# Starting addresses of four pairs of moving operands, relative to the stationary ones, in a fused attention and two-MLP kernel

## The chip, the cores and the metric

The kernel runs on one core of a Trainium2 chip. The metric is the device time of one execution in microseconds (us). Each core has a TensorE for matrix products (PE in the profile, with its weight loads shown apart as PEld), a VectorE (DVE), a ScalarE (ACT), a GpSimd (POOL) and queues that issue DMAs (SP is the one used most here). All of them work out of an on-chip memory with 128 partitions; products land in a second memory with banks of 512 float32 columns per partition.

## The reference

Three blocks follow each other, with B = 2, N = 6016, C = 256:

```python
qn = q / (norm(q, axis=1) + 1e-6);  kn = k / (norm(k, axis=1) + 1e-6)
a = softmax(kn.transpose(0, 2, 1) @ qn / tau)          # 256 x 256 per batch
x = (v @ a).reshape(12032, 256)
x = (sigmoid(x @ w_gate) * (x @ w_val)) @ w_out        # width 1536
h = x @ w_in2
out = (h - tanh(h)) @ w_out2                           # width 2048
```

## The kernel before, in words

The first stage forms the 256 x 256 products of k and q over 47 blocks of 128 rows for each batch (`gram_chunk`, line 778 is its matmul), the softmax, and then folds the attention matrix into `w_gate` and `w_val`, so that v is multiplied with the folded weights and v @ a never appears by itself. Batch 0 is folded at the start (`fold_first`), batch 1 in the middle, during the one tile called SWITCH.

The second stage works through 24 tiles of tokens, 12 for each batch: 22 of 512 columns, and two (SWITCH and LAST) of 384. All operands are held transposed, so tokens are columns. Each float32 product is made of three passes with operands split in two halves named hi and lo (`product3`, line 752): w_hi with x_lo, w_lo with x_hi, w_hi with x_hi. Each pass is one weight load of 128 columns (the stationary operand, a slice of the weights) and one matmul (the moving operand, 512 or 384 columns of activations). The moving operands are four pairs:

- `vt_hi`, `vt_lo`: v transposed. `U(j)` multiplies them with `gate_w` and `val_w`: 12 matmuls for each of the J1 = 12 chunks.
- `g1_hi`, `g1_lo`: the gated product of chunk j, in 3 slots. `D(t, j)` multiplies them with `out_w`: 6 matmuls.
- `x2_hi`, `x2_lo`: the output of the first MLP. `P_(t, i)` multiplies them with `in2_w`: 6 matmuls for each of J2 = 16 chunks.
- `g2_hi`, `g2_lo`: h - tanh(h) of chunk i, in 3 slots. `O(t, i)` multiplies them with `out2_w`: 6 matmuls.

`body(t)` writes out the order on TensorE by hand: U(2) D(0) U(3) D(1) and so on up to U(11) D(9), then D(10), U(12) (which is U(0) of the next tile), D(11), U(13), then P(0) to P(3), O(0), P(4), O(1), up to P(15) O(12), and O(13) to O(15). In that order there are 49 places in a usual tile at which the moving pair changes. Waits before each step ask for product banks (`free_bank`) and for the halves (`g_lo_made`, `x2_lo_made`, `vt_lo_made`).

For each chunk ScalarE reads the bank and writes `func_out` (line 444), VectorE makes `product` (line 642 or 645), ScalarE rounds it into the hi half (line 452), and VectorE subtracts for the lo half (line 651). The vt halves come from lines 427 and 627, the x2 halves from lines 436 and 634. GpSimd splits the weights into halves at the start and once more, for gate and val, around the SWITCH tile.

`sb` allocates memory in order, each tensor at the next multiple of 32 bytes. All weights, and everything allocated before and between the four moving pairs, has a size per partition that is a multiple of 512 bytes. The slice of weights that one load reads is 128 float32, which is 512 bytes, and begins at such a multiple. So in this kernel every moving operand and every stationary operand of `product3` begins at the same place modulo 512 bytes. A 512-column moving operand reads 2048 bytes per partition.

Of the kernel before, what the change touches and what calls it, by code (L numbers as in the profile page):

```python
# [7 lines left out]
def attn_two_mlp_kernel(  # L8
# [32 lines left out]
    F32, F32R = mybir.dt.float32, mybir.dt.float32r  # L41
# [3 lines left out]
    P = 128  # L45
    B, N, C = q.shape
    KC = C // P
    J1 = w_gate.shape[1] // P
    J2 = w2_in.shape[1] // P
    T = 512  # L50
# [6 lines left out]
    SLOTS = 3  # L57
# [61 lines left out]
        return nth(t, ("U", J1 - 2 + AHEAD[tile] + i // 2), tile)  # L119

    with ExitStack() as ctx:
        def sb(name, shape, dt=F32, stack=ctx):
            return stack.enter_context(nc.sbuf_tensor(name, shape, dt))

        def sem(name):
            return ctx.enter_context(nc.semaphore(name))


        def pair(name, shape, stack=ctx):
            return sb(name + "_hi", shape, F32R, stack), sb(name + "_lo", shape, F32R, stack)  # L130

        gate_hi, gate_lo = pair("gate_w", [P, KC, J1 * P])
        val_hi, val_lo = pair("val_w", [P, KC, J1 * P])
        wout_hi, wout_lo = pair("out_w", [P, J1, C])
        win_hi, win_lo = pair("in2_w", [P, KC, J2 * P])
        wout2_hi, wout2_lo = pair("out2_w", [P, J2, C])
        att = sb("att", [P, KC, C])
        att_t_hi, att_t_lo = pair("att_t", [P, KC, C])
        ident = sb("ident", [P, P])
        ones = sb("ones", [P, P])  # L140
        v_in = sb("v_in", [P, KC, TB, Q])
# [21 lines left out]

        func_out = sb("func_out", [P, 2, T])
        product = sb("product", [P, 2, T])
        vt_hi, vt_lo = pair("vt", [P, KC, T])
        g1_hi, g1_lo = pair("g1", [P, SLOTS, T])
        x2_hi, x2_lo = pair("x2", [P, KC, T])
        g2_hi, g2_lo = pair("g2", [P, SLOTS, T])
        tau_inv = sb("tau_inv", [P, 2])  # L170


# [787 lines left out]
```

## Time and profile before

| | us |
|---|---|
| median of 2 runs | 2354.19 |
| those runs | 2353.77 and 2354.61 |
| profiled execution, its own time | 2354.47 |
| its span, first to last instruction | 2352.7 |

TensorE is at work for 98% of the span and its weight loads for 82%, VectorE 50%, ScalarE 40%, GpSimd 4%. In 38 of 40 slices the clock that TensorE was granted is at 9 tenths or more of full speed, as a mean 0.994. In the profile a matmul's duration overlaps that of the next one, since matmuls are pipelined. How fast TensorE really works is therefore read from the distance between the starts of two matmuls, called the pitch below. The printed starts are rounded to 0.01 us, so a pitch is taken over several matmuls.

### The profile page before, as it was taken

The page shows a single profiled execution, that of the slowest core. Times are in us where ns is not written, and L with a number is a line of the kernel's source. Part 1 is how long each engine was busy: PE and PEld are TensorE (multiplying, and loading weights), DVE is VectorE, ACT ScalarE, POOL GpSimd, SP SyncE. Part 2 cuts the span into 40 slices and gives each one's busy share as a digit, 9 for nine tenths or more (in the row PEclk, how much of TensorE's full clock was granted, in tenths as well). Part 3 has the DMA queues.
Part 4 walks back from the last instruction along what each step waited for, and adds up shares of the span by engine and source line. Part 5 has one row for each costly group of instructions (what it writes and reads, how often), then busy time and mean ns, then how long its engine had stood idle before and what let it go on. Part 6 is the DMA issues. An engine that isn't in the chain of part 4 may idle for free.

```text
span 2352.7 us, 28301 instructions
## 1 busy us (share of the span) xinstructions
PE 2310.6 (98%) x10332; PEld 1935.0 (82%) x10332; DVE 1166.5 (50%) x1643; ACT 935.6 (40%) x1550; POOL 105.3 (4%) x76
## 2 busy tenths in 40 slices
PE   8899999999999999999989999999999999999998
PEld 6678888888888888888888888888888888888888
DVE  6975445445354454454554544544545445445454
ACT  4544334344344343343433433434434434334343
POOL 3450000000000000000030000000000000000000
PEclk9899999999999999999999999999999999999999
DMA  8720100100100001001110010010010000100000
GB/s 294 234 63 10 18 9 9 18 9 9 18 9 9 9 9 18 9 7 18 27 45 9 8 18 9 9 18 9 9 18 9 9 10 8 18 9 7 9 9 8
DMA packets 211649, 61.81 MB, mean 26 GB/s; under 512 B 200224, under 2 KB 200480, under 8 KB 211616
## 3 DMA queue, kind: packets, MB, share of 16 engines
q1 hardware_dynamic: 208304, 49.31, 9.4%
q0 software_dynamic: 3312, 12.06, 1.7%
q8 instruction: 20, 0.33, 0.1%
q14 instruction: 13, 0.11, 0.0%
HBM read 49.02 MB, written 12.32 MB: 26 GB/s over the span
## 4 chain that ended last, share of the span: by engine, by line
PE 93%; issue 2%; DVE 2%; POOL 1%; SPq 1%; ACT 1%; DMA 1%; DVEq 0%; ACTq 0%
PE up L752 54%; PE acc L752 22%; PE x_acc L752 17%; DMA qk_in<-in_k 1%; DVE sq_sum L536 1%; POOL in_w_lo L382 0%; PE x_acc L778 0%; POOL out_w_lo L382 0%; SPq L304 0%; DVE g_lo L651 0%; SPq L294 0%; ACT squares L399 0%; POOL in_w_hi L380 0%; DVE vt_lo L627 0%; POOL out_w_hi L380 0%
## 5 line engine op out<-in xcount | busy, mean ns | idle before, releaser
L444 ACT ACTIVATE func_out<-up 128x512 f32<-128x512 f32 (+1 forms) x672 | 396.1, 589 | 827.8 <-PE up L752 827.5
L651 DVE TENSOR_TENSOR g_lo<-product,g_hi 128x512 fp32r<-128x512 f32 (+1 forms) x672 | 470.7, 701 | 391.8 <-ACT g_hi L452 389.4
L452 ACT ACTIVATE g_hi<-product 128x512 fp32r<-128x512 f32 (+1 forms) x672 | 418.5, 623 | 442.2 <-PE acc L752 216.2
L642 DVE TENSOR_TENSOR product<-up,func_out 128x512 f32<-128x512 f32 (+1 forms) x288 | 196.2, 681 | 455.1 <-ACT func_out L444 454.8
L645 DVE TENSOR_TENSOR product<-up,func_out 128x512 f32<-128x512 f32 (+1 forms) x384 | 261.2, 680 | 183.7 <-ACT func_out L444 174.8
L752 PE MATMUL up<-x_lo,in_w_hi 128*128 128x512 f32 (+1 forms) x768 | 296.6, 386 | 1.0 <-DVE x_lo L634 1.0
L752 PE MATMUL up<-x_hi,in_w_lo 128*128 128x512 f32 (+1 forms) x768 | 296.1, 386 | 0.0
L752 PE MATMUL up<-x_hi,in_w_hi 128*128 128x512 f32 (+1 forms) x768 | 296.0, 385 | 0.0
L752 PE MATMUL acc<-g_hi,out_w_hi 128*128 128x512 f32 (+1 forms) x768 | 295.4, 385 | 0.0
L752 PE MATMUL acc<-g_lo,out_w_hi 128*128 128x512 f32 (+1 forms) x768 | 295.4, 385 | 0.0
L752 PE MATMUL acc<-g_hi,out_w_lo 128*128 128x512 f32 (+1 forms) x768 | 295.3, 385 | 0.0
L752 PE MATMUL x_acc<-g_lo,out_w_hi 128*128 128x512 f32 (+1 forms) x576 | 222.3, 386 | 6.4 <-DVE g_lo L651 6.4
L752 PE MATMUL up<-vt_lo,gate_w_hi 128*128 128x512 f32 (+1 forms) x576 | 222.8, 387 | 5.7 <-issue 3.3
L752 PE MATMUL up<-vt_hi,gate_w_hi 128*128 128x512 f32 (+1 forms) x576 | 222.5, 386 | 0.0
L752 PE MATMUL up<-vt_hi,gate_w_lo 128*128 128x512 f32 (+1 forms) x576 | 222.5, 386 | 0.0
L752 PE MATMUL up<-vt_lo,val_w_hi 128*128 128x512 f32 (+1 forms) x576 | 222.1, 386 | 0.0
L752 PE MATMUL up<-vt_hi,val_w_hi 128*128 128x512 f32 (+1 forms) x576 | 222.0, 385 | 0.0
L752 PE MATMUL up<-vt_hi,val_w_lo 128*128 128x512 f32 (+1 forms) x576 | 222.0, 385 | 0.0
L752 PE MATMUL x_acc<-g_hi,out_w_hi 128*128 128x512 f32 (+1 forms) x576 | 221.9, 385 | 0.0
L752 PE MATMUL x_acc<-g_hi,out_w_lo 128*128 128x512 f32 (+1 forms) x576 | 221.9, 385 | 0.0
L752 PEld LDWEIGHTS up<-x_lo,in_w_hi 128*128 128x128 f32 x768 | 144.7, 188 | 29.6 <-issue 1.8
L752 PEld LDWEIGHTS up<-x_hi,in_w_lo 128*128 128x128 f32 x768 | 144.8, 189 | 27.5
(122 smaller groups left out, 2307.7 us busy)
## 6 DMA issues: line engine op xcount, KB each, us to landing
v_in<-in_v SPq DMA_DIRECT2D x176, 64.0 KB, 2.2
out_rows<-out_sb SPq DMA_DIRECT2D x176, 64.0 KB, 1.8
qk_in<-in_q SPq DMA_DIRECT2D x29, 384.0 KB, 4.1
qk_in<-in_k SPq DMA_DIRECT2D x29, 384.0 KB, 5.4
w_stage<-in_moe_w_out POOLq DMA_DIRECT2D x4, 512.0 KB, 4.4
w_stage<-in_moe_w_gate POOLq DMA_DIRECT2D x3, 512.0 KB, 5.1
out_sb<-in_moe_w_val POOLq DMA_DIRECT2D x3, 512.0 KB, 4.4
out_sb<-in_moe_w_out POOLq DMA_DIRECT2D x3, 512.0 KB, 4.3
```

The source lines that it names most:

```text
L444: act.activation(func_out[:, half, cut], src[:, cut], func).then_inc(func_made, 1)
L452: act.activation(hi[:, i % SLOTS, cut], product[:, half, cut], ACT.Copy).then_inc(g_hi_made, 1)
L536: dve.tensor_tensor(sq_sum[:, which, 0:size, :], sq_sum[:, which, 0:size, :], squares[:, which, 0:size, :], ALU.add).then_inc(sq_added, 1)
L642: dve.tensor_tensor(product[:, half, cut], up[2 * (i % 2) + 1][:, cut], func_out[:, half, cut], ALU.mult).then_inc(prod_made, 1)
L645: dve.tensor_tensor(product[:, half, cut], up[i % 4][:, cut], func_out[:, half, cut], ALU.subtract).then_inc(prod_made, 1)
L651: dve.tensor_tensor(lo[:, i % SLOTS, cut], product[:, half, cut], hi[:, i % SLOTS, cut].bitcast(F32), ALU.subtract).then_inc(g_lo_made, 1)
L752: mm = pe.matmul(psum, a, b, start=start and n == 0, stop=stop and n == 2, skip_group_check=shared_bank)
```

## The change

The allocator helper takes an alignment, small pads are allocated ahead of the four pairs, and three of the pairs are placed with an alignment of 4 bytes. No instruction is added, removed or moved.

```diff
-        def sb(name, shape, dt=F32, stack=ctx):
-            return stack.enter_context(nc.sbuf_tensor(name, shape, dt))
+        def sb(name, shape, dt=F32, stack=ctx, align=32):
+            return stack.enter_context(nc.sbuf_tensor(name, shape, dt, align_bytes=align))
...
-        def pair(name, shape, stack=ctx):
-            return sb(name + "_hi", shape, F32R, stack), sb(name + "_lo", shape, F32R, stack)
+        def pair(name, shape, stack=ctx, align=32):
+            return (sb(name + "_hi", shape, F32R, stack, align),
+                    sb(name + "_lo", shape, F32R, stack, align))
...
         product = sb("product", [P, 2, T])
-        vt_hi, vt_lo = pair("vt", [P, KC, T])
-        g1_hi, g1_lo = pair("g1", [P, SLOTS, T])
+        sb("pad_vt", [P, 2])
+        vt_hi, vt_lo = pair("vt", [P, KC, T], align=4)
+        sb("pad_g1", [P, 2], align=4)
+        g1_hi, g1_lo = pair("g1", [P, SLOTS, T], align=4)
+        sb("pad_x2", [P, 44], align=4)
         x2_hi, x2_lo = pair("x2", [P, KC, T])
-        g2_hi, g2_lo = pair("g2", [P, SLOTS, T])
+        sb("pad_g2", [P, 81])
+        g2_hi, g2_lo = pair("g2", [P, SLOTS, T], align=4)
         tau_inv = sb("tau_inv", [P, 2])
```

The pads are 8, 8, 176 and 324 bytes. Both halves of vt then begin 8 bytes past a multiple of 512, both of g1 16 bytes, both of x2 192 bytes, and both of g2 4 bytes (192 + 324 = 516). The weights stay where they were.

## Rows read from the trace of the kernel before

**Rows 1.** The page: busy time of each engine, share of the span, instructions.

```profile
PE 2310.6 (98%) x10332; PEld 1935.0 (82%) x10332; DVE 1166.5 (50%) x1643; ACT 935.6 (40%) x1550; POOL 105.3 (4%) x76
```

**Rows 2.** Waits of PE: who was waited for, us in total, times, longest.

```profile
PE acc L787 <- DVE expd L556: 12.7, 1, 12.7
...
PE x_acc L752 <- DVE g_lo L651: 6.4, 3, 5.5
```

**Rows 3.** Windows, PE: stretch, length, busy (matmuls), granted clock, DMA share, GB/s.

```profile
143.00:145.00 2.00, 2.00 (x6) 0.50 0.93 256
500.00:600.00 100.00, 100.00 (x443) 1.00 0.06 10
```

**Rows 4.** Groups by form, PE: count, busy us, mean ns, idle before.

```profile
L752 PE MATMUL up<-x_hi,in_w_lo 128*128 128x512 f32 x704 | 274.0, 389 | 0.0
...
L752 PE MATMUL up<-vt_hi,gate_w_hi 128*128 128x512 f32 x536 | 209.1, 390 | 0.0
...
L752 PE MATMUL x_acc<-g_hi,out_w_hi 128*128 128x512 f32 x528 | 205.5, 389 | 0.0
...
L752 PE MATMUL up<-x_hi,in_w_lo 128*128 128x384 f32 x64 | 22.1, 345 | 0.0
```

**Rows 5.** Timeline of PEld in a usual tile: start us, duration us.

```profile
1003.43 0.19 PEld L752 LDWEIGHTS x_acc<-g_hi,out_w_lo 128*128 128x128 f32 x1
```

**Rows 6.** Timeline of PE in the same stretch: first of six matmuls, and the seventh.

```profile
1003.43 0.39 PE L752 MATMUL x_acc<-g_lo,out_w_hi 128*128 128x512 f32 x1
...
1004.79 0.39 PE L752 MATMUL up<-vt_lo,gate_w_hi 128*128 128x512 f32 x1
```

**Rows 7.** Timeline of PE in the LAST tile: first of six, and the seventh.

```profile
2290.00 0.33 PE L752 MATMUL x_acc<-g_lo,out_w_hi 128*128 128x384 f32 x1
...
2291.04 0.34 PE L752 MATMUL up<-vt_lo,gate_w_hi 128*128 128x384 f32 x1
```

**Rows 8.** Timeline of PE at the start of the second stage: three pitches apart.

```profile
143.46 0.63 PE L752 MATMUL up<-vt_hi,gate_w_hi 128*128 128x512 f32 x1
...
144.74 0.63 PE L752 MATMUL up<-vt_hi,gate_w_hi 128*128 128x512 f32 x1
```

**Rows 9.** Timeline of PE in the first stage, then its group in 73 to 88.

```profile
74.75 12.47 PE L778 MATMUL x_acc<-qk_in 128*128 128x256 f32 x57
```

```profile
L778 PE MATMUL x_acc<-qk_in 128*128 128x256 f32 x69 | 15.5, 387 | 0.0
```

**Rows 10.** Timeline of PE around a fold in SWITCH: 12 matmuls of 512 columns.

```profile
1210.38 0.39 PE L752 MATMUL x_acc<-gate_w_lo,att_t_hi 128*128 128x512 f32 x1
...
1211.77 0.39 PE L752 MATMUL x_acc<-gate_w_lo,att_t_hi 128*128 128x512 f32 x1
...
1212.47 0.39 PE L752 MATMUL x_acc<-gate_w_lo,att_t_hi 128*128 128x512 f32 x1
...
1213.15 0.33 PE L752 MATMUL up<-x_lo,in_w_hi 128*128 128x384 f32 x1
```

**Rows 11.** Timeline of PE at a step from 512 to 384 columns, SWITCH.

```profile
1161.19 0.33 PE L752 MATMUL up<-vt_lo,gate_w_hi 128*128 128x384 f32 x1
...
1162.26 0.33 PE L752 MATMUL up<-vt_lo,val_w_hi 128*128 128x384 f32 x1
...
1163.30 0.33 PE L752 MATMUL x_acc<-g_lo,out_w_hi 128*128 128x384 f32 x1
```

**Rows 12.** Groups by form of the engines that write the pairs.

```profile
L651 DVE TENSOR_TENSOR g_lo<-product,g_hi 128x512 fp32r<-128x512 f32 x620 | 434.4, 701 | 365.6 <-ACT g_hi L452 363.3
L452 ACT ACTIVATE g_hi<-product 128x512 fp32r<-128x512 f32 x620 | 391.1, 631 | 405.4 <-PE acc L752 216.2 <-PE x_acc L752 132.1 <-DVE product L642 47.7
L444 ACT ACTIVATE func_out<-up 128x512 f32<-128x512 f32 x620 | 370.5, 598 | 780.1 <-PE up L752 780.1
...
L645 DVE TENSOR_TENSOR product<-up,func_out 128x512 f32<-128x512 f32 x352 | 243.4, 692 | 172.4 <-ACT func_out L444 164.4
```

## Prediction

> **What bounds the kernel now.** I began with the page's busy times: TensorE is busy for 2310.6 of 2352.7 us, and no other engine for more than half [rows 1]. The waits of TensorE come next: the longest is 12.7 us, once, in the first stage, and the longest of the second stage is 6.4 us in 3 waits [rows 2]. So about 2.2 ms are an unbroken stream of matmuls, and only their pitch, the distance from start to start, can move the time by much. A busy share near 100% does not tell whether that pitch is good, since a matmul's duration of 389 ns [rows 4] overlaps that of its neighbours.
>
> The pitch comes from windows and timelines. From 500 to 600 us 443 matmuls touch a stretch of 100 us at a granted clock of 1.00 [rows 3]; with the 0.39 us of one added for the edges that is 100.39 / 443 = 226.6 ns. Six matmuls in a row take 1004.79 - 1003.43 = 1.36 us, 226.7 ns each [rows 6]. At 2.4 GHz this is 544 cycles for 512 columns: 32 more than the columns need. With 384 columns six take 1.04 us [rows 7], 173.3 ns or 416 cycles: again 32 more. So the surcharge is a fixed 13.3 ns for each matmul, independent of its length.
>
> Three places bear on what the surcharge is. At the start of the second stage the granted clock is 0.50, the 1.2 GHz level [rows 3], and three pitches take 1.28 us [rows 8]: 426.7 ns, exactly 512 cycles of that clock, with no surcharge. In the first stage 57 matmuls of plain float32 take 12.47 us, less one duration of 0.387 over 56 pitches: 215.8 ns for 256 columns at full clock [rows 9]. That is two cycles per column and only some 2.5 ns more. So where the moving operand is taken in at half the rate, in either way, the surcharge is gone. And in the second stage the load of the next weights begins together with the running matmul (both stand at 1003.43, [rows 5, 6]) and takes 188 ns of the 227: the two reads of the memory run side by side, beginning at the same place modulo 512.
>
> A fourth place shows that the surcharge depends on something that moves. After a step from 384 to 512 columns the first six matmuls of a fold take 1211.77 - 1210.38 = 1.39 us, 231.7 ns each; the last three 0.68 us, 226.7 each [rows 10]. After a step from 512 to 384 the first six take 1.07 us, 178 ns, and the next six 1.04, 173.3 [rows 11]. The reads fall out of step with each other, cost more, and fall back into the same pattern.
>
> **The change part by part.** It moves only addresses. The number of instructions and their order stay. Three things could be priced.
>
> *The matmuls of `product3`.* Of 512 columns there are six groups of 704, six of 536 and three of 528, of which one each stands in [rows 4]: 4224 + 3216 + 1584 = 9024. Of 384 columns there are 6 x 64 (one stands there), 6 x 40 and 3 x 48 = 768. Together 9792. For each of the 9792 the change alters the distance between the moving operand and the weights being loaded beside it. If the surcharge is the meeting of two reads that walk through the same places at the same time, a distance of 8, 16, 192 or 4 bytes parts them. No matmul of the kernel before has such a distance, so the price is bounded from both sides. From below: no surcharge at all, 213.3 ns, which saves 13.4 x 9792 = 131 us. The nearest row with a weight load beside each matmul and nothing lost to it is the first stage's 215.8 [rows 9]; that saves 226.7 - 215.8 = 10.9 ns for each, 9792 x 10.9 = 107 us. Nothing is the middle bound: 0 us. From above: every matmul stays as dear as the first six of a fold, 231.7 [rows 10], which adds 5.0 x 9792 = 49 us. I take 215.8, because both rows in which the two reads do not press on each other, at either clock, show almost no surcharge.
>
> A rule speaks against this. The Trainium skill, "SBUF — State Buffer" (section "SBUF: two separate sides") and "TensorE: Matmul & The Clock Gate" (section "Step-by-step: what each phase is for"), says that TensorE has two independent read ports and that loading the next weights takes nothing from the running matmul; by that the change gives 0 us. The same page on TensorE (section "Back-to-back issue gap") gives N / 2.4 + 2.5 ns, 215.8 for 512 columns, which the first stage meets and the second misses by 11 ns, so the trace does not follow it where the rate is full.
>
> *The folds.* Their stationary operand is `att_t` and their moving one is the weights; neither is moved. Their 144 matmuls keep their cost: 0 us.
>
> *The writers of the four pairs.* ScalarE and VectorE now write and read at places that are not multiples of 32. For a chunk of the second MLP (P and O, 12 matmuls, 2.72 us now and 2.59 at 215.8) ScalarE works 598 + 631 ns and VectorE 692 + 701 ns [rows 12]. From below the cost is nothing; were the two that touch a pair twice as slow, ScalarE would need 1.86 and VectorE 2.09 us, still under 2.59. What hides it is the matmul stream itself. Without that cover, at the few places where PE waits for g_lo, 6.4 us in 3 waits [rows 2], it could cost some 3 x 1.3 = 4 us. I take 0. There is no gain either, since nothing there is shortened that PE waits for.
>
> The sum, against the profiled execution's 2354.5 us: 2354.5 - 107 = 2247.5, so 2248 us. The profiled execution is 0.3 us above the median of the runs, which changes nothing. Late next would still be TensorE: its columns alone take 9024 x 213.3 + 768 x 160 ns = 2048 us. Both other engines stay under 60% busy.
>
> **The rivals.**
>
> *Nothing moves (2354 us).* The surcharge is a price of having a second reader at all, or of changing weights at full rate, wherever the operands lie. For it: it is exactly 32 cycles for both lengths and for each of the four pairs, and after each disturbance it comes back to that figure, as if a lag between the two reads took up any distance by itself. The two ports of the skill would end here too. Against it: during those disturbances the price changes, with the same instructions.
>
> *Only some distances help (about 2300 us).* 16 and 192 bytes are whole groups of four float32, 8 and 4 are not, and the operands at 8 and 4 then straddle such groups. If only g1 and x2 gain: 72 + 96 of 408 matmuls of a tile, 41%, 44 us, 2310. If only vt and g2 gain: 144 + 96 of 408, 59%, 63 us, 2291. For it: only that the four are different. Against: no row shows any of these cases.
>
> *Each change of the pair disturbs the stream (slower).* The mechanism is the one seen behind a change of length. With one place for all, going from U to D or from P to O leaves the two reads in step. With four places each of the 49 changes in a tile shifts one against the other. A disturbance over six matmuls costs 1.39 - 1.36 = 0.03 us and over twelve 1213.15 - 1210.38 - 2.72 = 0.05 us [rows 10]. Per tile that is 37 x 0.03 + 12 x 0.05 = 1.7 us, times 24 is 41 us: 2395 us, 1.7% slower. It decides in favour of slower by over 2% when a disturbance does not settle within the six matmuls of D, P and O: all at 231.7 gives 2403. The dearest six matmuls in a row that I read set that figure. For it: the disturbances are there and always repeat. Against: they follow a change of length, and whether a change of place does the same is not shown.
>
> The Trainium skill, "SBUF — State Buffer" (section "Specifications (TRN2)"), gives lines of 16 bytes and a penalty for each crossing into a new one. An operand at 8 or 4 bytes past a line touches 129 lines instead of 128. No run here shows such a penalty; by this rule alone the change would lose a little.
>
> As a mechanism of this kernel that has its own bound: one more cycle for each of the 240 x 24 = 5760 matmuls on vt and g2 is 5760 x 0.42 ns = 2.4 us, which is within 2% and counted with the first rival.
>
> **How the numbers follow.** The full gain, around 2248, has 0.30. Only some distances help: 0.16, of which 0.12 ends over 2% (below 2307) and 0.04 within. Nothing moves: 0.28. Disturbances: 0.26, of which 0.08 stays within 2% (up to 2401) and 0.18 beyond. So faster 0.42, same 0.40, slower 0.18, where 2% is also about what a measurement of this kernel can tell from no change. The likeliest case's own range is 2223 (no surcharge at all) to 2265 (a sixth of the gain lost). The range for 8 in 10 has to hold the cases of both signs: from 2235, halfway to the bound of 2223 that the first stage's row doesn't reach, up to 2405, just past the full disturbance. That leaves out about 0.03 below and 0.15 above.
>
> **What the profile of the changed kernel would show.** The window from 500 to 600 us should have some 465 matmuls instead of 443 at a granted clock of 1.00. Six matmuls in a row should take 1.29 to 1.30 us. Durations of 389 ns should fall to about 378. The weight loads should still begin with the matmul beside them. The folds should keep their 12-matmul pattern, and the writers' means should be within a few ns of [rows 12]. If only some distances help, the pitch differs between the U, D, P and O runs, and that names which. If disturbances come, the first matmuls after each change of pair are dearer than the later ones. The prediction is wrong if a pitch of 226.7 stays in all four, or if it grows anywhere.

## The result: 2417 us, 2.7% slower

| | before | after |
|---|---|---|
| median of 2 runs, us | 2354.19 | 2417.19 |
| span of the profiled execution, us | 2352.7 | 2413.8 |
| ratio, 95% interval | | 1.0268 (1.0223 to 1.0312) |

The forecast was 2248 us in a range of 2235 to 2405, with 0.18 on slower by over 2%. The time is above the range.

The waits of TensorE after (who was waited for, us in total, times, longest) answer to [rows 2]:

```profile
PE x_acc L783 <- DMA qk_in<-in_k: 12.5, 7, 3.4
PE x_acc L757 <- DVE g_lo L656: 6.4, 2, 6.2
PE acc L792 <- DVE expd L561: 3.6, 1, 3.6
```

There is no new wait in the second stage. The window that answers to [rows 3] (stretch, length, busy and matmuls, granted clock, DMA share, GB/s):

```profile
500.00:600.00 100.00, 100.00 (x429) 1.00 0.06 10
```

At the same granted clock of 1.00, 429 matmuls touch the stretch instead of 443: 100.4 / 429 = 234.0 ns each instead of 226.6. So the loss is in the pitch. The timeline of TensorE in a usual tile gives it by kind, as [rows 6] did before. The first and second rows below are 12 matmuls of U apart, the second and third 12 of D, the fourth and fifth the 24 of P(0) to P(3), and the last two 6 of O:

```profile
557.41 0.39 PE L757 MATMUL up<-vt_lo,gate_w_hi 128*128 128x512 f32 x1
...
560.20 0.40 PE L757 MATMUL x_acc<-g_lo,out_w_hi 128*128 128x512 f32 x1
...
562.99 0.39 PE L757 MATMUL up<-vt_lo,gate_w_hi 128*128 128x512 f32 x1
...
569.96 0.40 PE L757 MATMUL up<-x_lo,in_w_hi 128*128 128x512 f32 x1
...
575.56 0.40 PE L757 MATMUL acc<-g_lo,out_w_hi 128*128 128x512 f32 x1
...
576.98 0.40 PE L757 MATMUL up<-x_lo,in_w_hi 128*128 128x512 f32 x1
```

These are 2.79 us / 12 = 232.5 for U, 2.79 / 12 = 232.5 for D, 5.60 / 24 = 233.3 for P and 1.42 / 6 = 237 ns for O. None of the four gained; all four lost, and not by the same amount. Means over all matmuls of 512 columns, from the starts in the trace (pauses of 300 ns and more left out):

| kind, pair | bytes past | before, ns | after, ns |
|---|---|---|---|
| U, vt | 8 | 226.7 | 232.9 |
| D, g1 | 16 | 226.7 | 231.6 |
| P, x2 | 192 | 226.7 | 233.4 |
| O, g2 | 4 | 226.6 | 237.5 |
| all | | 226.7 | 233.9 |

7.2 ns on 9024 matmuls are 65 us, and the matmuls of 384 columns add some 2.5 us by the same reckoning. Set against that are 6.4 us less in three waits, two of them of the first stage: for DVE expd 12.7 fell to 3.6 and for issue 3.3 to 1.7, for the DMA of k 8.2 rose to 12.5. 67.4 - 6.4 = 61.0, and the spans differ by 61.1 us.

The writers of the pairs did not change; these two groups by form (count, busy us, mean ns, idle before) answer to [rows 12], where they took 631 and 701 ns:

```profile
L457 ACT ACTIVATE g_hi<-product 128x512 fp32r<-128x512 f32 x620 | 391.4, 631 | 424.1 <-PE acc L757 241.9 <-PE x_acc L757 132.1 <-DVE product L647 49.7
...
L656 DVE TENSOR_TENSOR g_lo<-product,g_hi 128x512 fp32r<-128x512 f32 x620 | 433.1, 699 | 384.8 <-ACT g_hi L457 384.8
```

### The profile page after: what moved, and what is told of

It is laid out like the page before. It is cut to its first block, busy times and chain, and to the rows that moved or that the text cites. A ratio compares the mean times of both kernels' runs of the same rounds, so it can differ in the third digit from the quotient of the medians.

```text
span 2413.8 us, 28301 instructions
## 1 busy us (share of the span) xinstructions
PE 2377.9 (99%) x10332; PEld 1949.1 (81%) x10332; DVE 1157.6 (48%) x1643; ACT 936.2 (39%) x1550; POOL 105.8 (4%) x76
## 4 chain that ended last, share of the span: by engine, by line
PE 94%; DVE 1%; POOL 1%; issue 1%; SPq 1%; ACT 0%; DMA 0%; DVEq 0%; ACTq 0%
PE up L757 55%; PE acc L757 22%; PE x_acc L757 17%; PE x_acc L783 1%; DVE sq_sum L541 1%; POOL in_w_lo L387 0%; DMA qk_in<-in_k 0%; POOL out_w_lo L387 0%; SPq L309 0%; ACT squares L404 0%; SPq L299 0%; POOL in_w_hi L385 0%; POOL out_w_hi L385 0%; DVE vt_lo L632 0%; DVE g_lo L656 0%
## 5 line engine op out<-in xcount | busy, mean ns | idle before, releaser
L757 PE MATMUL acc<-g_lo,out_w_hi 128*128 128x512 f32 (+1 forms) x768 | 303.4, 395 | 0.0
L757 PE MATMUL acc<-g_hi,out_w_hi 128*128 128x512 f32 (+1 forms) x768 | 303.2, 395 | 0.0
L757 PE MATMUL acc<-g_hi,out_w_lo 128*128 128x512 f32 (+1 forms) x768 | 302.9, 394 | 0.0
L757 PE MATMUL up<-x_lo,in_w_hi 128*128 128x512 f32 (+1 forms) x768 | 301.5, 393 | 1.0 <-DVE x_lo L639 1.0
L757 PE MATMUL x_acc<-g_lo,out_w_hi 128*128 128x512 f32 (+1 forms) x576 | 226.6, 393 | 6.4 <-DVE g_lo L656 6.4
L757 PEld LDWEIGHTS acc<-g_hi,out_w_hi 128*128 128x128 f32 x768 | 144.2, 188 | 35.0
L757 PEld LDWEIGHTS acc<-g_lo,out_w_hi 128*128 128x128 f32 x768 | 144.4, 188 | 34.8
```

The source lines that it names most:

```text
L757: mm = pe.matmul(psum, a, b, start=start and n == 0, stop=stop and n == 2, skip_group_check=shared_bank)
```

## The experiments

float32r is the type of the hi and lo halves (F32R in the kernel). In the tables a pitch is the mean from start to start in the trace. "Settled" is the mean over the last twelve pitches of a stream.

### Standing price or disturbance: one pair alone, and all at one place

Two theories could give the slower time. A: each place has a price that stands as long as it is used. B: only a change from one place to another disturbs the stream, as the third rival of the prediction had it.

`g2_alone` is the kernel before with one pad:

```diff
+        sb("pad_g2", [P, 1], align=4)
-        g2_hi, g2_lo = pair("g2", [P, SLOTS, T])
+        g2_hi, g2_lo = pair("g2", [P, SLOTS, T], align=4)
```

> The kernel before with one pair moved: g2 begins 4 bytes past a multiple of 512, vt, g1 and x2 stay at 0. Theory A (each distance between moving operand and weights has a standing price, whatever the neighbours do): the O matmuls have the pitch of the changed kernel, 237.5 ns, the U, D and P matmuls stay at 226.7; 96 x 24 = 2304 matmuls by 10.8 ns are 25 us, so 2379 us. Theory B (each change of place disturbs the stream): the P runs beside the O runs are disturbed as much as they are, both 230 to 237 ns, and the long run of P(0) to P(3) settles at 226.7; some 2390 us or more. U and D stay at 226.7 in both.

Measured: 2375.4 us, ratio 1.0117 (1.0096 to 1.0139). U and D stay at 226.7. The kernel before had a median of 2349.05 us beside it, so the 25 us of theory A lead to 2374. The timeline in the second half of a tile, P(0) to P(3), then O(0), then P(4):

```profile
563.22 0.39 PE L754 MATMUL up<-x_lo,in_w_hi 128*128 128x512 f32 x1
...
568.66 0.40 PE L754 MATMUL acc<-g_lo,out_w_hi 128*128 128x512 f32 x1
...
570.08 0.39 PE L754 MATMUL up<-x_lo,in_w_hi 128*128 128x512 f32 x1
...
571.47 0.39 PE L754 MATMUL acc<-g_lo,out_w_hi 128*128 128x512 f32 x1
```

The long run of P is at 5.44 / 24 = 226.7. O(0), at the new place, is at 1.42 / 6 = 237, and P(4), whose own place is unchanged, at 1.39 / 6 = 232. Both theories hold a part: the place has a price, and here a change of place disturbs the next run. In the means over this kernel O is at 235.3 and all P at 230.6. The six pitches of P between two O runs are 231.7, 233.3, 235.8, 224.2, 230.8, 235.9 ns. The six folds of SWITCH [rows 10] begin, in their mean read from the trace, with 229.8, 233.3, 235.7, 224.3, 230.7, 235.8: almost the same pattern, behind a change of length instead of a change of place.

`all_4` and `all_16` give all four pairs one place, 4 or 16 bytes past a multiple of 512. That leaves no change of place from run to run:

```diff
+        sb("pad_vt", [P, 1], align=4)      # all_16: [P, 4]
+        vt_hi, vt_lo = pair("vt", [P, KC, T], align=4)
+        g1_hi, g1_lo = pair("g1", [P, SLOTS, T], align=4)
+        x2_hi, x2_lo = pair("x2", [P, KC, T], align=4)
+        g2_hi, g2_lo = pair("g2", [P, SLOTS, T], align=4)
```

> All four pairs begin 4 bytes past a multiple of 512, so nothing changes its place from run to run. Theory A: all four kinds at about 237.5 ns, 9792 x 10.8 ns = 106 us more than before, 2460 us. Theory B: all at 226.7, 2354 us.

> All four pairs begin 16 bytes past a multiple of 512. Theory A: all four kinds near the pitch that D has in the changed kernel, 230 to 232 ns, 2354 + 9792 x 4.8 ns = 2401 us; if a shift of 16 bytes is in truth free and D was only disturbed by its neighbour, 226.7 or less. Theory B: 226.7, 2354 us.

Measured, one execution each: 2445 us and 2396 us, where the kernel before had a median of 2349 us beside them, with executions from 2343 to 2353. The pitch is 236.9 ns for `all_4` in all four kinds (236.8 to 237.0) and 231.7 for `all_16` in all four. So theory A carries the main part, and theory B alone, which gave no change here, is out. The 2460 us of theory A for `all_4` come down to 2444, against 2445 measured, by three terms: the kernel before took 5.4 us less here than 2354.5, the pitch is 0.6 ns lower (6 us), and the 768 matmuls of 384 columns went only from 173.8 to 178.2 ns, not up by 10.8 (5 us). The 2401 us for `all_16` come down to 2396 by the first of them alone.

### The price of every place

`scan_4b` measures the disputed price by itself. It computes nothing of the reference. Its core, with the start and stop marks left out:

```python
def group(psum, o, groups=12):
    for g in range(groups):
        for n, (a, b) in enumerate(((w_hi, m_lo), (w_lo, m_hi), (w_hi, m_hi))):
            pe.matmul(psum, a[:, (g % 11) * 128:(g % 11 + 1) * 128], b[:, o:o + 512], ...)
for o in range(128):            # 4 bytes each
    group(odd if o % 2 == 0 else even, o)
```

> A kernel of its own that leaves out the whole computation: one stream of 36 matmuls of 512 float32r columns for each of 128 distances, 0, 4, 8 up to 508 bytes, between the start of the moving operand and that of the weights modulo 512, with a weight load of 128 columns for each matmul, in the same order of hi and lo. Theory A: the pitch is a function of the distance, 226.7 ns at 0, about 237 at 4, 233 at 8, 231 at 16 and 233 at 192 bytes, and there may be distances below 226.7, down to 215.8. Theory B: 226.7 at every distance once the first six matmuls are over.

The timeline of TensorE at 4 and at 16 bytes, twelve matmuls apart each:

```profile
33.43 0.40 PE L60 MATMUL even<-m_hi,w_hi 128*128 128x512 f32 x1
...
36.27 0.40 PE L60 MATMUL even<-m_hi,w_hi 128*128 128x512 f32 x1
...
58.47 0.39 PE L60 MATMUL odd<-m_hi,w_hi 128*128 128x512 f32 x1
...
61.25 0.39 PE L60 MATMUL odd<-m_hi,w_hi 128*128 128x512 f32 x1
```

2.84 / 12 = 236.7 ns and 2.78 / 12 = 231.7 ns. All settled pitches:

| bytes past | settled ns | the kind at that place in the changed kernel |
|---|---|---|
| 0 | 226.7 | (all four before) |
| 4 | 236.7 | O 237.5 |
| 8 | 233.3 | U 232.9 |
| 12 | 228.8 | |
| 16 | 231.7 | D 231.6 |
| 20 | 240.0 (the highest) | |
| 28, 60, 156, 236, 240, 252 | 226.7 | |
| 192 | 233.3 | P 233.4 |
| mean of all 128 places | 232.9 | |

Three things follow. The four prices of the changed kernel are, within 0.8 ns, those of four of these places. No place lies below 226.7, where the kernel before already was. And the second half of the scan, 256 to 508 bytes, repeats the first to within 0.1 ns, so in this scan the place counts modulo 256, not 512. Each of these values was reached from one predecessor only, the place 4 bytes before. Within 16 bytes the means are 232.0 at 0, 237.0 at 4, 233.3 at 8 and 229.2 at 12. Of the 128 values 88 lie at 226.7 or a multiple of 3.3 ns above it, which is 8 cycles at 2.4 GHz.

`places` takes the weights too through 16 places, 0 to 60 bytes, with streams of 24 matmuls:

> A kernel of its own that leaves out the whole computation: streams of 24 matmuls of 512 float32r columns with the weights at 16 places, 0, 4 up to 60 bytes past a multiple of 512, and for each of them the moving operand at the same 16 places. If nothing but the meeting of two reads made the surcharge, some pair of places would be free of it, 215.8 ns or 213.3. If 32 cycles are a floor of the kind of matmul, no pair goes below 226.7 for a settled stream, and 226.7 is reached by some pairs for every place of the weights. If only the distance counts, each row of 16 is the first one shifted.

The lowest settled pitch of the 256 pairs is again 226.7. Fourteen of the 16 places of the weights have some place of the moving operand that reaches it, the other two stop at 228.3. The rows are not one row shifted: with the moving operand at 0, weights at 0 give 226.7, weights at 4 to 60 bytes give 230.0 to 233.3; the dear place at 4 bytes is dear for nearly every place of the weights (230.0 to 240.0). So both places count, and the distance by itself is not the right variable. The moving one counts more: the sixteen places of the weights have means of 232.0 to 232.9, those of the moving operand 227.9 to 236.8. A cheaper pair than the one before was not found.

### What the floor of 226.7 is made of

`cases` varies the load of the weights, the length, which half is moved, and the type:

> A kernel of its own that leaves out the whole computation: streams of 36 matmuls, one stream for each case. First the weight load has 128, 96, 64 or 32 columns, at distances of 0, 4 and 16 bytes. Theory C (each line of weights read costs the moving stream a cycle): the surcharge over 512 columns falls with the load, 32, 24, 16, 8 cycles at distance 0, so 226.7, 223.3, 220.0, 216.7 ns. Rival D (a fixed price for changing weights): 226.7 for all four. Then lengths of 384, 256 and 128 columns: both 173.3, 120.0 and 66.7 ns at distance 0, unless the load itself is longer than that. Then the weights begin 4, 8, 16 or 192 bytes late and the moving operand at the distances 0, 4, 8, 16, 60 and 192 bytes from them: if only the distance counts, each row repeats the scan, 226.7, 236.7, 233.3, 231.7, 226.7, 233.3; if the places themselves count, it doesn't. Then only the hi or only the lo half moved: between the scan's value and 226.7. Then plain float32, 256 columns: 215.8 ns at every distance. Then bfloat16: by theory C a smaller surcharge than 13.3 ns, since the same columns are half as many bytes, and by rival D the same.

| case, 512 columns unless said | settled ns |
|---|---|
| 0 bytes, loads of 128, 96, 64, 32 columns | 226.7, 230.4, 229.6, 231.8 |
| 4 bytes, the same | 236.8, 235.4, 234.4, 236.7 |
| 384 and 256 columns, 0 bytes | 173.3, 120.0 |
| 384 and 256 columns, 4 bytes | 173.3, 123.3 |
| 384 and 256 columns, 16 bytes | 175.5, 118.8 |
| 128 columns, 0, 4 and 16 bytes | 111.7 at each |
| only hi at 4, only lo at 4 bytes | 237.8, 233.3 |
| only hi at 16, only lo at 16 bytes | 231.2, 231.8 |
| only hi at 192, only lo at 192 bytes | 234.4, 228.8 |
| weights 192 late, moving 0, 4, 8, 16, 60, 192 bytes from them | 226.7, 236.7, 233.3, 231.7, 226.7, 233.1 |
| weights 4 late, the same | 237.8, 233.3, 233.3, 236.7, 233.2, 236.6 |
| weights 8 late, the same | 231.2, 228.9, 231.1, 231.2, 237.6, 230.6 |
| weights 16 late, the same | 233.3, 230.0, 233.3, 226.7, 229.9, 229.3 |
| plain float32, 256 columns, 0, 4, 8, 16, 192 bytes | 215.8 at each |
| bfloat16, at 0 and at 2, 4, 8, 16 bytes | 215.8, and 216.7, 215.8, 215.8, 215.8 |

Theory C, a cycle for each line of weights read, asked for 216.7 with a load of 32 columns; it was 231.8, though the profile's mean duration of a load fell from 188 to 108 ns. At 0 bytes the floor does not shrink with the load. Rival D, a fixed price for changing weights, asked for 226.7 with every load and for the same surcharge in bfloat16; the narrower loads cost 3 to 5 ns more, and bfloat16 has no such surcharge. The prices of the halves do not add up. At 4 bytes the hi half, used in two of three passes, costs 11.1 ns by itself and the lo half 6.6, while both together cost 10.0. Of the three types tried only float32r shows the 13.3 ns and more than 1 ns of dependence on the place. Plain float32, which takes two cycles a column, and bfloat16, which has half the bytes, do not. (A matmul of plain float32 in the program stands as two records in the trace, 72 for 36, so 215.8 ns is half the cost of one.)

Three things in the table were not expected. The weights 192 bytes late repeat the scan, those 4, 8 and 16 late do not. With 128 columns the pitch is 111.7 ns at each place where 66.7 were expected, so something other than the columns sets it there, and no run shows what. And with 256 columns 0 bytes is not the cheapest place. The timeline at 16 bytes has 24 matmuls between these rows:

```profile
161.61 0.28 PE L81 MATMUL even<-m_hi,w_hi 128*128 128x256 f32 x1
...
164.46 0.28 PE L81 MATMUL even<-m_hi,w_hi 128*128 128x256 f32 x1
```

2.85 / 24 = 118.8 ns, against 120.0 at 0 bytes. That is 1% and 29 cycles above the columns' own time instead of 32.

`reads` changes how the moving operand is read, with the same number of columns:

```diff
+ every second:   m[:, o:o + 1024:2]
+ one element:    m[:, o:o + 1].to_broadcast([P, 512])
+ four elements:  m[:, o:o + 4].unsqueeze(1).to_broadcast([P, 128, 4])
```

> A kernel of its own that leaves out the whole computation: streams of 36 float32r matmuls of 512 columns at 0, 4 and 16 bytes whose moving operand is read in four ways: one element after the other, every second element (twice the bytes passed over), the same element 512 times, and the same four elements 128 times; then weights with every second element, and with one element 128 times. If the floor of 226.7 ns and what lies above it come from reading the moving operand through the memory at full rate, the two repeated forms drop to 215.8 ns and lose their dependence on the distance, and every second element is much dearer. If they belong to the product itself (float32r at full rate), all forms stay at 226.7 for distance 0. If the load of the weights takes part, every second element of the weights changes the pitch and the repeated one lowers it; if it doesn't, both stay at 226.7, 236.7 and 231.7.

The timeline for four elements 128 times at 0 bytes, twelve matmuls apart (2.60 / 12 = 216.7 ns), and the settled pitches of all:

```profile
63.73 0.38 PE L87 MATMUL even<-m_hi,w_hi 128*128 128x512 f32 x1
...
66.33 0.38 PE L87 MATMUL even<-m_hi,w_hi 128*128 128x512 f32 x1
```

| moving operand, weights | 0 bytes | 4 bytes | 16 bytes |
|---|---|---|---|
| in order, in order | 226.7 | 236.7 | 231.7 |
| every second element, in order | 453.3 | 453.3 | 453.3 |
| one element 512 times, in order | 216.7 | 216.7 | 216.7 |
| four elements 128 times, in order | 216.7 | 217.2 | 216.7 |
| in order, every second element | 233.4 | 233.4 | 233.7 |
| in order, one element 128 times | 231.6 | 236.8 | 228.9 |

With the same product, the same weights and the same number of columns, an operand that is read again and again from one place costs 216.7 ns and its place no longer matters. One that passes over twice the bytes costs exactly twice the floor. So the surcharge belongs to drawing the moving operand out of memory at full rate. The reads of the weights take part in it, in both directions. Read otherwise, they raise the pitch at 0 bytes to 231.6 or 233.4. At 4 bytes every second element lowers it from 236.7 to 233.4, and at 16 bytes one element 128 times lowers it from 231.7 to 228.9. In `cases` a load of 64 columns lowered it at 4 bytes from 236.8 to 234.4. So the prediction was right that the two reads act on each other. Its cause falls because no form, width or place of the weights brings 512 columns below 226.7. Every matmul of every run has a load beside it, so what the pitch would be without one is not shown.

### One place, several patterns

A place of 240 bytes was at the floor in the scan. `all_240` puts all four pairs there, `four_floor` puts vt, g1, x2 and g2 at 28, 60, 156 and 236:

> The kernel before with all four pairs 240 bytes past a multiple of 512, a distance that the scan has at 226.7 ns. Theory A (the price is the scan's function of the distance): 226.7 ns in all four kinds, no change, ratio 1.000. A rival, that only a distance of 0 is cheap in the whole kernel, because engines other than TensorE use the pairs too: above 226.7, slower by 1% or more.

> Four different distances, each of which the scan has at 226.7 ns: vt 28, g1 60, x2 156 and g2 236 bytes. If only the standing price of a distance counted, this is 226.7 ns everywhere and no change, 2354 us. If a change of place disturbs the stream besides, as the P runs beside the moved O runs suggest (231.9 ns instead of 226.7), the six-matmul runs of D, P and O lie near 230 to 232 ns and the start of the U runs too: 49 changes per tile by 0.02 to 0.03 us by 24 tiles are 24 to 35 us, about 2385 us.

`all_240` took 2428 us, ratio 1.0368 (1.0335 to 1.0402). Its four executions lie at 2403, 2441, 2429 and 2427 us, at nearly the same mean clock (0.993 to 0.996) and much farther apart than those of the other kernels. Against the 2347.8 us of the kernel before they are 2.3 to 4.0% slower, so the interval is narrower than the spread. The windows of the profiled one, which is the fastest, point to a reason:

```profile
500.00:600.00 100.00, 100.00 (x443) 1.00 0.06 10
1000.00:1100.00 100.00, 100.00 (x443) 1.00 0.06 9
...
1300.00:1400.00 100.00, 100.00 (x424) 1.00 0.07 11
1700.00:1800.00 100.00, 100.00 (x424) 1.00 0.06 10
```

The first batch runs at 226.7 ns, and behind the SWITCH tile, with the same instructions and the same places, the second at 100.4 / 424 = 236.8, from its first matmuls at 1252.7 us on. Between them lie the SWITCH tile's matmuls of 384 columns, at about 180 ns where the kernel before has 173.5, and the folds. An execution wholly in the dear pattern would take about 9792 x 10 ns = 98 us more than the 2348 of before, 2446. The slowest took 2441, which fits, but the three slower ones have no trace, so that they ran longer in the dear pattern is not shown. My rival, that 0 alone is cheap because other engines touch the pairs, named the time (slower by over 1%) but not the cause: the first batch shows 226.7 with all engines at work.

`history` tests that by itself. It reaches six places from each of several predecessors:

> A kernel of its own that leaves out the whole computation: streams of 36 float32r matmuls at the distances 0, 4, 8, 16, 192 and 240 bytes, each reached from every one of these, from 128 bytes, and from plain float32 matmuls. If the pitch is a function of the distance alone, each has one value whatever came before. If a distance has several patterns into which the stream can fall, as 231.7 ns for 240 bytes in the kernel against 226.7 in the scan suggests, 240 has two or more, and 0, which came back to 226.7 behind every disturbance of the kernel before, has one.

| place | settled pitch, reached from 0, 4, 8, 16, 192, 240, 128 bytes and from plain float32 |
|---|---|
| 0 | 226.7 from all |
| 4 | 236.7 from all |
| 8 | 233.3 from all |
| 16 | 231.7 from all |
| 192 | 233.3 from all |
| 240 | 233.3, 236.7, 226.7, 233.3, 236.7, 236.7, 233.3, 236.7 |

The prediction's place (0) and the four of the change each have one value, whatever came before. 240 bytes has three (128 bytes, seen as a predecessor, also has several, 231.7 to 233.3), and in other parts of the same stream 4 and 16 bytes led to other ones of the three (226.7 and 236.7), so not even the last predecessor decides it alone. So a low value in a scan is worth something only where it comes back from every predecessor. The scan's other places at 226.7 (28, 60, 156, 236 and 252 bytes) were not tried in this way.

`four_floor` took 2357 us, ratio 1.0036 (1.0019 to 1.0053): its pitch is 227.8 in the mean. U, D and O are at 227.9, 227.4 and 226.9, and P at 228.8. Each kind comes back to 226.7, so what is left are disturbances. They cost 1.1 ns a matmul, 11 us, not the 31 us that I expected of them from the fold's rows. Not all of them come from a change of place. P behind O begins with 228.3, 230.0, 233.3 and 227.5 ns. In the long run P(0) to P(3), where the place stays, the seventh to tenth pitches are 229.2, 230.0, 233.4 and 227.5, and the same comes again from the thirteenth and the nineteenth. So P is disturbed at every new chunk, with or without a change of place, and these pitches don't tell how much the change itself adds. In the kernel before no new chunk disturbs anything.

### One part undone

`g2_back` is the changed kernel with g2 at 0 again (pad of 80 instead of 81 elements):

> The changed kernel with one part undone: g2 is back at 0, vt, g1 and x2 stay at 8, 16 and 192 bytes. By the standing prices the O matmuls fall from 237.5 to between 226.7 (settled) and about 231 ns (disturbed by the P runs beside them): 2304 matmuls by 6 to 11 ns are 15 to 25 us less than the changed kernel, so 2392 to 2402 us, and 1.6 to 2.1% above the kernel before. If O's place had nothing to do with it, 2417 stays.

Measured: 2395.8 us, ratio 1.0211 (1.0178 to 1.0245), where the changed kernel had 1.0268. O falls from 237.5 to 229.4 in the mean; the O runs behind each other at a tile's end are at 226.7, those between P runs at 230.0 (227.0, 235.0, 228.9, 232.3, 229.9, 227.0). U, D and P keep 232.7, 231.7 and 233.3. The mean over all goes from 233.9 to 231.9, 2.0 ns by 9792 or 19 us, in the expected 15 to 25. The times alone don't separate the two kernels: the ratios differ by 0.0057, some 13 us, and their intervals (1.0178 to 1.0245 and 1.0223 to 1.0312) overlap. The pitches of O carry this result.

## Why the prediction was wrong

**The bound was right.** TensorE's stream sets the time, the pitch is what the change moves, and no other engine or wait took part in the second stage. The writers cost nothing, as forecast, and the 144 matmuls of the folds kept theirs within 0.2 us.

**The step that failed is the price of the 9792 matmuls.** I took the 13.3 ns above the columns' own time for a meeting of two reads that walk in step, which a distance would part, and chose 215.8 ns for it. The measured price is 233.9 in the mean. The settled pitch of 512 columns was never below 226.7, at any of the 128 places of the scan nor the 256 pairs of places. The term was to be -107 us and was +67. Two readings led there. First, the surcharge vanished at half the rate [rows 8, 9]. That was right, but it speaks for any cost of reading at full rate, and `reads` ties it to the moving operand's own reading: 216.7 ns when the operand is repeated, 226.7 when it passes by. The load of the weights shifts the price of a place by a few ns, but no place, width or form of it took the surcharge away. Second, all four pairs began in step with the weights, and I took this for the dear case. For 512 columns it is the cheapest of the six places that `history` tried: 0 gives 226.7 from every predecessor, and the 128 places average 232.9.

**A row had said so.** The disturbed pitches of [rows 10, 11] were all the evidence that the trace had of operands out of step, and they were dearer in the mean, 231.7 against 226.7. I listed them as a rival and set the price by a row of another kind of matmul instead. A term for which the trace has rows on one side only should have leaned to that side.

**The rivals.** "Nothing moves" had the floor right: there are 32 cycles that no place tried removes from 512 columns. It had the rest wrong. "Only some distances help" is out for 512 columns: none of 128 helps. The rival on the other side gave 2395 to 2403 us. Its disturbances exist (`g2_alone`), but four different cheap places cost only 9 us in all (`four_floor`, 2357 us). What it lacked is a price that stands: `all_4` and `all_16` have no change of place between runs and lose 4.1% and 2.0%. The upper bound of 231.7 ns was the dearest mean of six that I had read, and it was taken for the worst that could be. The trace of before had dearer ones. Six pitches in folds of the first stage, at a granted clock of 1.00, average 233.2 ns from 101.47 us on and 232.5 from 106.84 on, and with them the same sum gives 2418 and 2411. The scan's worst is 240.0. The bound set too low put the top of the range, 2405, below the 2417 that came.

**The rules of the Trainium skill.** The sum does not need them. The Trainium skill, "SBUF — State Buffer" (section "SBUF: two separate sides") gives TensorE a second, independent read port for the load of weights. The runs agree in so far as no load changed the floor of 226.7 ns downwards, and disagree in that its place, width and form move the pitch: up by 2.9 to 6.7 ns with the moving operand at 0 bytes, and down by as much as 6.7 with it at 4 bytes (230.0 with the weights at 52). The Trainium skill, same page, "Specifications (TRN2)", has a penalty for each crossing into a new line of 16 bytes. By that rule 4, 8 and 12 bytes into a line would cost alike, since each touches one line more than 0. The scan has 237.0, 233.3 and 229.2 ns in the mean, against 232.0 at 0, so the rule does not give these prices. The 2.5 ns above the columns' own time that the Trainium skill, "TensorE: Matmul & The Clock Gate" (section "Back-to-back issue gap"), gives for a matmul by itself fit plain float32 and bfloat16, 215.8, and not float32r.

**Open.** How the memory produces 8-cycle steps, why 4 bytes is dear and 12 cheap, and what holds the floor at 32 cycles for 384 and 512 columns when 256 columns went to 29 at 16 bytes, was not settled. Nor was why 384 columns at 4 bytes take 173.3 ns in `cases` and 178.2 in `all_4`. No run shows the memory's own arbitration.

## What to carry to other kernels

For float32r matmuls of 384 or 512 columns at full clock, begin moving and stationary operands at multiples of 512 bytes, all of them, and check the pitch: 226.7 ns for 512 columns is the best that any run here reached with operands that are read in order, and a place of the moving operand taken at random costs 2.7% of the stream on average. A price seen to vanish under lighter load is not shown to be avoidable under full load; and where the trace has a disturbed stretch, look for the dearest one in the whole trace before it is taken as a bound. When scanning for a place, reach each one from several others, because some hold more than one pattern.

## What the runs showed of the hardware that I had not expected

- The pitch of a float32r matmul of 512 columns depends on where its operands begin, from 226.7 to 240.0 ns over places 4 bytes apart, in a pattern that repeats every 256 bytes, while plain float32 (256 columns, per record) stays at 215.8 and bfloat16 at 215.8 to 216.7 at every place tried.
- Reading one line again and again brings float32r to 216.7 ns; reading every second element doubles it to 453.3.
- At 0 bytes a narrower load of weights does not shorten the pitch: 226.7 ns with 128 columns, 231.8 with 32. At 4 and 16 bytes the form of the load moves it down as well: 231.7 ns to 228.9 with one element repeated at 16 bytes.
- The same instructions at the same places can run at 226.7 ns for a millisecond and at 236.7 for the next (`all_240`, either side of the SWITCH tile).
